# Batch-by-batch keys, choices and digits for the first routing round of a retention, MoE and GLU kernel

## The chip, the cores and the metric

The program runs on one core of one Trainium2 chip. The metric is the device time of one execution in microseconds (us); several executions are timed and the median is taken. The engines of the core work side by side and meet only at semaphores: TensorE (PE, with its weight loads shown apart as PEld), VectorE (DVE), ScalarE (ACT), GpSimd (POOL) and SyncE (SP), which issues the DMA transfers. Each of them takes its own instructions strictly in order.

## The reference

Three layers follow one another. The first is a retention layer over 4 batches, 8 heads, 768 steps and head size 64:

```python
for t in range(S):
    state = gamma[None, :, None, None] * state + np.einsum('bhd,bhe->bhde', k[:, :, t], v[:, :, t])
    y[:, :, t] = scale * np.einsum('bhd,bhde->bhe', q[:, :, t], state)
```

Its output is 3072 tokens of 512 numbers. The second layer sends each token to one of 8 experts with a capacity of 384 tokens each. All logits (token, expert) are walked from the largest down; a token goes to the expert of the first logit whose expert still has room:

```python
logits = x @ w_gate
order = np.argsort(-logits.flatten())
for idx in order:
    tok, e = (int(idx) // E, int(idx) % E)
    if assigned[tok] >= 0 or counts[e] >= cap:
        continue
    assigned[tok] = e
    counts[e] += 1
for e in range(E):
    mask = assigned == e
    h = np.maximum(x[mask] @ w1[e], 0.0)
    out[mask] = h @ w2[e]
```

The third layer is a gated unit on all tokens: `(sigmoid(x @ w_gate) * (x @ w_val)) @ w_out`.

## The kernel before

**Tiling.** The tokens of a batch are cut into C = 6 tiles of 128 (one per partition), so there are U = 24 units, numbered u = 6b + c. The attention part runs as a software pipeline over steps s = 0 to 28. In step s, unit s-1 has q and k transposed (PE lines 648 and 655), unit s-2 its scores made (636) and masked by DVE (`att`, 572), unit s-3 its output and state products (684, 688, 698) and DVE's scaling into `xTa` (584) and the running `state` (594, 597), unit s-4 its partial logits (668) and DVE's transposition into `xrow` (563), and unit s-5 its logits finished on PE (623) and copied by DVE into column u of `logits` (554). Steps 0 to 5 and 24 to 28 are written out; steps 6 to 23 are a hardware loop over b = 1, 2, 3 with six steps in its body, so step s has b = s // 6 and c = s % 6.

**Who waits for whom in a step.** PE's products of line 668 in step s wait until DVE has made the copy of unit s-5, since both use the bank `ps_l`. They are the first thing on PE in a step that needs DVE work of that same step. DVE's `xTa` waits for the products of line 688. ACT copies the transposed q, k and the partial logits (`qT`, `kT`, `lparts`, lines 518, 523, 531).

**The queue of SP.** In step s SP issues the loads of q and k for unit s+5 and of v for unit s+3, and then four stores of `xrow` for unit s-4. From step 19 on four loads of resident weights stand behind each step's stores. From step 21 on ACT has `high` (line 282) for three resident tiles behind each step's copies; the first of a group of four waits until its four loads have landed.

**After the attention.** DVE waits for all logits and then prepares the first routing round: `prepare(True)` finds for each token the best logit (`best`), turns it into a sortable integer (`bits`, `key`), finds the expert it belongs to (`wide`, `top`, `choice`) and cuts the key into seven digits of five bits (`digit_i`, `digit_f`). The arrays have one column per unit. Then a radix search alternates DVE and PE in seven visits (`compare_first`, `first_threshold`), the chosen tokens are numbered, their row numbers go to GpSimd's gather, and the expert rounds begin. Each later round's routing is done beside the matmuls of the round before it.

**Waits within DVE.** `link(ins)` lets DVE wait until ins has written its result; `count_only(ins)` counts it on the same semaphore (`dve_chain`) and goes on at once. `PREP_CHAIN` and `CHAIN_START` are where the count stands before the first round.

Of the kernel before, what the change touches and what calls it, by code (L numbers as in the profile page):

```python
# [8 lines left out]
I32 = mybir.dt.int32  # L9
U32 = mybir.dt.uint32  # L10
ALU = mybir.AluOpType
ACT = mybir.ActivationFunctionType
AX_X = mybir.AxisListType.X
P = 128


def retention_moe_glu_kernel(nc, q, k, v, w_router, w1, w2, w_gate, w_val, w_out, decay, out):
# [15 lines left out]
    with ctx:  # L33
# [21 lines left out]
        BIG = 1.0e6  # L55
        PREP_CHAIN = 13
        FIRST_CHAIN = 79
        ROUTE_CHAIN = 125
        CHAIN_START = PREP_CHAIN
        TABLES = 8 + 5 + 3 + 3  # L60
# [226 lines left out]
        if True:  # L287
# [251 lines left out]

            def attend_vector(dve):  # L540
                nc.vector.memset(state[:, :, :, :], 0.0).then_inc(state_cleared, 1)
# [7 lines left out]
                def body(b, c, s):  # L549
# [25 lines left out]
                    if alive(s, 3):  # L575
# [10 lines left out]
                        if cc < C - 1:  # L586
# [3 lines left out]
                            for half in range(2):  # L590
# [4 lines left out]
                                else:  # L595

                                    ins = nc.vector.tensor_tensor(state[rows, new, :, rows], fresh_kv,
                                                                  state[rows, cc % 2, :, rows], ALU.add)
                                ins.then_inc(state_ready, 1)

                slots(dve, body, 0, U + 4)
# [294 lines left out]
        def _(dve):  # L896
            attend_vector(dve)

            link_count = [0]
# [73 lines left out]

            def prepare(first):
                prepare_keys()
                prepare_digits(first)

# [10 lines left out]

            def prepare_digits(first):

# [6 lines left out]
                link(nc.vector.tensor_scalar(digit_f[:, :, :], digit_i[:, :, :], 1.0, None, ALU.add))  # L997
                if first:
                    compare_first(digit_f[:, 0, :])
                else:  # L1000
                    compare(digit_f[:, 0, :])
                raise_by(digit_f[:, 0, :], 1)
# [164 lines left out]
            def one_round(i, follows):  # L1167
# [21 lines left out]
                def prepare_next():  # L1189

                    if vis[0] == VISITS + 1 and follows:
                        close()
                        prepare_keys()
                        vis[0] += 1
                    elif vis[0] == VISITS + 2 and follows:
                        prepare_digits(False)
                        vis[0] += 1
# [35 lines left out]
                out_rows(i)  # L1233

            dve.sem_inc(orow_ready, TT)
            dve.sem_inc(orow_free, 1)
            dve.wait_ge(tables_made, TABLES)
# [8 lines left out]
            close()  # L1246
            prepare(False)
            assert link_count[0] == FIRST_CHAIN, link_count[0]
# [224 lines left out]
```

## Time and profile before

| what | us |
|---|---|
| median of 3 executions | 1080.89 |
| lowest and highest of them | 1080.59, 1082.13 |
| the profiled execution, its own time | 1084.76 |
| span of the profiled execution, from its first to its last instruction | 1082.7 |
| PE busy in the span | 1027.4 |
| DVE busy in the span | 697.5 |

Times in rows are microseconds from the start of the span. The granted clock (PEclk) is 1.00 at TensorE's 2.4 GHz and 0.50 at 1.2 GHz. A note in brackets behind a row is the idle time of that engine before it and what ended it.

### The profile page before, as it was taken

To read this page: it belongs to the slowest core of one execution; us is meant where nothing else is said; L and a number is where in the kernel's file an instruction comes from. 1 tells how busy PE (TensorE), PEld (TensorE's weight loads), DVE (VectorE), ACT (ScalarE), POOL (GpSimd) and SP (SyncE) were. 2 spreads that over 40 slices of the span, in tenths; PEclk is the share of its full clock that TensorE was granted. 3 is DMA by queue.
4 is the path that set the end of the run, shared out by engine and by line. 5 is a ranking of instruction groups with operands and counts; after the bars stand their busy time and mean duration, and the time that the engine had idled before them with its cause. 6 is when DMAs were issued, how large, how long until landed. Compare 5 with 4: busy or idle time off the path is not lost.

```text
span 1082.7 us, 20008 instructions
## 1 busy us (share of the span) xinstructions
PE 1027.4 (95%) x7130; PEld 958.4 (89%) x7130; DVE 697.5 (64%) x1880; ACT 330.0 (30%) x630; POOL 116.6 (11%) x141
## 2 busy tenths in 40 slices
PE   8999734999999999999999999999999999999996
PEld 7888623999999999999999999999999999999995
DVE  4777578777577657766776677666775677554211
ACT  3222423422333233322332333233412341234110
POOL 4212601033000101010100010011001100110001
PEclk9999865999999999999999999999999999999998
DMA  8899843403241324122322332132314231323000
GB/s 197 202 222 229 224 137 117 119 29 93 74 146 40 88 78 128 59 83 83 110 77 59 107 108 79 49 117 92 95 39 127 80 107 38 119 78 117 1 1 30
DMA packets 197356, 107.69 MB, mean 99 GB/s; under 512 B 81936, under 2 KB 182800, under 8 KB 197264
## 3 DMA queue, kind: packets, MB, share of 16 engines
q1 hardware_dynamic: 193424, 93.94, 31.2%
q0 software_dynamic: 3840, 12.59, 3.6%
q8 instruction: 50, 0.82, 0.3%
q14 instruction: 42, 0.34, 0.1%
HBM read 88.41 MB, written 18.09 MB: 98 GB/s over the span
## 4 chain that ended last, share of the span: by engine, by line
PE 93%; DVE 2%; DMA 1%; issue 1%; SPq 1%; ACT 0%; POOL 0%; DVEq 0%; POOLq 0%; ACTq 0%
PE bank L1323 21%; PE bank L1325 21%; PE bank L1324 21%; PE bank L1416 6%; PE bank L1417 6%; PE bank L1415 6%; PE bank L636 2%; PE bank L688 2%; PE bank L684 2%; PE bank L648 1%; PE bank L1277 1%; PE bank L655 1%; PE bank L698 1%; PE bank L668 1%; PE bank L610 1%
## 5 line engine op out<-in xcount | busy, mean ns | idle before, releaser
L1323 PE MATMUL bank<-h2h,resident 128*128 128x384 f32 x768 | 261.2, 340 | 0.0
L1325 PE MATMUL bank<-h2h,resident 128*128 128x384 f32 x768 | 257.9, 336 | 0.0
L1324 PE MATMUL bank<-h2l,resident 128*128 128x384 f32 x768 | 257.3, 335 | 0.0
L1323 PEld LDWEIGHTS bank<-h2h,resident 128*128 128x128 f32 x768 | 144.4, 188 | 2.9
L1324 PEld LDWEIGHTS bank<-h2l,resident 128*128 128x128 f32 x768 | 144.3, 188 | 2.9
L1325 PEld LDWEIGHTS bank<-h2h,resident 128*128 128x128 f32 x768 | 144.1, 188 | 0.0
L834 ACT ACTIVATE ring<-ring_raw 128x512 fp32r<-128x512 f32 x192 | 117.7, 624 | 61.7 <-DMA ring_raw<-in_moe_w_out_dram 42.0
L1150 DVE TENSOR_TENSOR pf<-bank,gate 128x384 f32<-128x384 f32 x96 | 53.5, 557 | 123.7 <-PE bank L1325 115.9
L858 ACT ACTIVATE ph<-pf 128x384 fp32r<-128x384 f32 x96 | 50.4, 525 | 252.1 <-DVE pf L1150 252.1
L1159 DVE TENSOR_TENSOR ring<-ring_raw,ring 128x512 fp32r<-128x512 f32 x192 | 126.0, 682 | 0.0
L854 ACT ACTIVATE gate<-bank 128x384 f32<-128x384 f32 x96 | 46.9, 489 | 145.9 <-PE bank L1325 145.8
L1154 DVE TENSOR_TENSOR pl<-pf,ph 128x384 fp32r<-128x384 f32 x96 | 54.2, 564 | 56.8 <-ACT ph L858 56.8
L1323 PE MATMUL bank<-xh,ring 128*128 128x384 f32 x256 | 88.4, 345 | 0.6 <-DVE xl L1140 0.6
L1323 PE MATMUL bank<-hh,ring 128*128 128x384 f32 x256 | 87.0, 340 | 0.0
L1324 PE MATMUL bank<-xl,ring 128*128 128x384 f32 x256 | 86.4, 337 | 0.0
L1325 PE MATMUL bank<-xh,ring 128*128 128x384 f32 x256 | 86.3, 337 | 0.0
L1324 PE MATMUL bank<-hl,ring 128*128 128x384 f32 x256 | 85.7, 335 | 0.0
L1325 PE MATMUL bank<-hh,ring 128*128 128x384 f32 x256 | 85.7, 335 | 0.0
L1417 PE MATMUL bank<-ring,pl 128*128 128x512 f32 x192 | 76.0, 396 | 0.0
L1416 PE MATMUL bank<-ring,ph 128*128 128x512 f32 x192 | 75.8, 395 | 0.0
L1415 PE MATMUL bank<-ring,ph 128*128 128x512 f32 x192 | 74.8, 390 | 0.2 <-issue 0.2
L791 POOL DMA_INDIRECT xg<-xrows,ids x24 | 23.4, 977 | 460.2 <-DVE ids L1111 419.1
(192 smaller groups left out, 1642.4 us busy)
## 6 DMA issues: line engine op xcount, KB each, us to landing
ring_raw<-in_moe_w_dram SPq DMA_DIRECT2D x128, 256.0 KB, 3.0
ring_raw<-in_moe_w_out_dram SPq DMA_DIRECT2D x64, 256.0 KB, 2.8
qraw<-in_q_dram SPq DMA_DIRECT2D x24, 256.0 KB, 3.3
kraw<-in_k_dram SPq DMA_DIRECT2D x24, 256.0 KB, 3.7
vraw<-in_v_dram SPq DMA_DIRECT2D x24, 256.0 KB, 4.2
xrows<-xrow SPq DMA_DIRECT2D x96, 64.0 KB, 2.3
xlaid<-xg SPq DMA_DIRECT2D x7, 768.0 KB, 4.4
zg<-xlaid SPq DMA_DIRECT2D x28, 192.0 KB, 4.2
```

The lines of the kernel that those rows point to most:

```text
L834: nc.scalar.activation(ring[:, n % RING, 0, :], ring_raw[n % RING][:, :], ACT.Copy).then_inc(piece_hi, 1)
L854: nc.scalar.activation(gate[:, f % 2, :], bank[2 * (f % 2)][:, 0:CAP], ACT.Sigmoid).then_inc(gate_ready, 1)
L858: nc.scalar.activation(ph[:, f % 2, :], pf[:, f % 2, :], ACT.Copy).then_inc(ph_ready, 1)
L1150: nc.vector.tensor_tensor(pf[:, f % 2, :], bank[2 * (f % 2) + 1][:, 0:CAP], gate[:, f % 2, :], ALU.mult).then_inc(p_ready, 1)
L1154: nc.vector.tensor_tensor(pl[:, f % 2, :], pf[:, f % 2, :], ph[:, f % 2, :].bitcast(F32), ALU.subtract).then_inc(pl_ready, 1)
L1159: nc.vector.tensor_tensor(ring[:, s, 1, :], ring_raw[s][:, :], ring[:, s, 0, :].bitcast(F32), ALU.subtract).then_inc(piece_lo, 1)
L1323: nc.tensor.matmul(ps, wh, xhi, start=start, stop=False)
L1324: nc.tensor.matmul(ps, wh, xlo, start=False, stop=False)
L1325: return nc.tensor.matmul(ps, wl, xhi, start=False, stop=stop)
L1415: nc.tensor.matmul(PS_OUT[j][:, :], ph[:, f % 2, toks], wh, start=f == 0, stop=False)
L1416: nc.tensor.matmul(PS_OUT[j][:, :], ph[:, f % 2, toks], wl, start=False, stop=False)
L1417: last = nc.tensor.matmul(PS_OUT[j][:, :], pl[:, f % 2, toks], wh, start=False, stop=False)
```

## The change

The keys, choices and digits of the first routing round are made in pieces of six columns. For the first three batches DVE makes them inside the attention loop: the six instructions of `first_keys` for batch b-1 stand at the end of the loop's step c = 4, the five of `first_digits` at the end of its step c = 5. Only the fourth batch's six columns remain behind the attention (`prepare_last`). The product of `top` with `unassigned`, which is all ones in the first round, is left out of the first round, so that 11 instructions per batch stand where 12 stood for all batches. Later rounds are prepared as before.

```diff
-        CHAIN_START = PREP_CHAIN
+        UNIT_CHAIN = 11
+        CHAIN_START = (U // C) * UNIT_CHAIN + 1
...
+                    if s is None and c >= C - 2:
+                        prepare_ahead(b, c - C + 2)
...
+            def first_keys(n):
+
+                tiles = bass.ds(n * C, C)
+                logged = masked[:, :, tiles]
+                link(nc.vector.reduce_max(best[:, tiles], over_experts(logged), AX_X))
+                count_only(nc.vector.tensor_scalar(bits[:, tiles], best[:, tiles], 0.0, None, ALU.add))
+                link(nc.vector.tensor_tensor(wide[:, :, tiles], logged, best[:, tiles].unsqueeze(1).to_broadcast([P, E, C]), ALU.is_equal))
+                count_only(nc.vector.tensor_scalar(key[:, tiles], bits[:, tiles].bitcast(I32), 31, -2147483648,
+                                                   ALU.arith_shift_right, ALU.bitwise_or))
+                link(nc.vector.tensor_tensor(wide[:, :, tiles], wide[:, :, tiles],
+                                             priority[:, :].unsqueeze(2).to_broadcast([P, E, C]), ALU.mult))
+                count_only(nc.vector.tensor_tensor(key[:, tiles], key[:, tiles], bits[:, tiles].bitcast(I32), ALU.bitwise_xor))
+
+            def first_digits(n):
+
+                tiles = bass.ds(n * C, C)
+                link(nc.vector.reduce_max(top[:, 0, tiles], over_experts(wide[:, :, tiles]), AX_X))
+                count_only(nc.vector.tensor_tensor(digit_i[:, :, tiles], key[:, tiles].unsqueeze(1).to_broadcast([P, DIGITS, C]),
+                                                   shift[:, :].unsqueeze(2).to_broadcast([P, DIGITS, C]), ALU.logical_shift_right))
+                link(nc.vector.tensor_tensor(choice[:, :, tiles], priority[:, :].unsqueeze(2).to_broadcast([P, E, C]),
+                                             top[:, 0, tiles].unsqueeze(1).to_broadcast([P, E, C]), ALU.is_equal))
+                link(nc.vector.tensor_scalar(digit_i[:, :, tiles], digit_i[:, :, tiles], RADIX - 1, None, ALU.bitwise_and))
+                link(nc.vector.tensor_scalar(digit_f[:, :, tiles], digit_i[:, :, tiles], 1.0, None, ALU.add))
+
+            def prepare_ahead(b, part):
+
+                link_base[0] = (b - 1) * UNIT_CHAIN
+                link_count[0] = 0 if part == 0 else 6
+                if part == 0:
+                    dve.wait_ge(tables_made, TABLES)
+                    dve.wait_ge(logits_saved, b * C)
+                    first_keys(b - 1)
...
+                else:
+                    first_digits(b - 1)
...
+            def prepare_last():
+
+                link_base[0] = 0
+                link_count[0] = (B - 1) * UNIT_CHAIN
+                first_keys(B - 1)
+                first_digits(B - 1)
+                compare_first(digit_f[:, 0, :])
+                raise_by(digit_f[:, 0, :], 1)
...
             dve.wait_ge(logits_saved, U)
-            prepare(True)
+            prepare_last()
```

On DVE, at the end of step c = 4 of the attention loop, the first instructions of `first_keys` come in behind the state update and ahead of the next step's copy of logits. REGISTER_ALU and ISA rows are work of the sequencer: addresses and the counts waited for, which depend on the loop's b.

```order
 L597 TENSOR_TENSOR state<-bank,state 64x4x64
+L978 ISA [waits logits_saved,tables_made]
+L978 TENSOR_REDUCE best<-logits 128x6
+L905 ISA
+L979 REGISTER_ALU [waits dve_chain]
+L979 TENSOR_SCALAR bits<-best 128x6
+L980 REGISTER_ALU
+L980 TENSOR_TENSOR wide<-logits,best 128x8x6
+L905 REGISTER_ALU
+L981 REGISTER_ALU [waits dve_chain]
```

The copy of logits (line 554) stood directly behind the state update; now six vector instructions stand between them. The same happens at the end of step c = 5, where the loop turns. Its last instructions and the branch are these:

```order
+L993 TENSOR_TENSOR choice<-priority,top 128x8x6
+L905 REGISTER_ALU
+L995 TENSOR_SCALAR digit_i<-digit_i 128x7x6 [waits dve_chain]
+L905 REGISTER_ALU
+L996 REGISTER_ALU [waits dve_chain]
+L996 TENSOR_SCALAR digit_f<-digit_i 128x7x6
+L905 REGISTER_ALU
+L358 REGISTER_ALU [waits dve_chain]
 L358 COMPARE_AND_BRANCH
 L554 COPY logits<-bank 128x8 [waits logits_done]
```

The branch now comes behind a wait for the last of the five new instructions. Behind the attention, DVE's preparation of the first round read so before:

```order
-L980 TENSOR_REDUCE best<-logits 128x24 [waits logits_saved,tables_made]
-L981 TENSOR_SCALAR bits<-best 128x24 [waits dve_chain]
-L982 TENSOR_TENSOR wide<-logits,best 128x192
-L984 TENSOR_SCALAR key<-bits 128x24 [waits dve_chain]
-L986 TENSOR_TENSOR wide<-wide,priority 128x192
-L987 TENSOR_TENSOR key<-key,bits 128x24 [waits dve_chain]
-L991 TENSOR_REDUCE top<-wide 128x24
-L992 TENSOR_TENSOR digit_i<-key,shift 128x168 [waits dve_chain]
-L994 TENSOR_TENSOR top<-top,unassigned 128x24
-L995 TENSOR_SCALAR digit_i<-digit_i 128x168 [waits dve_chain]
-L996 TENSOR_TENSOR choice<-priority,top 128x192
-L997 TENSOR_SCALAR digit_f<-digit_i 128x168 [waits dve_chain]
```

and reads so now, in the same place:

```order
+L978 TENSOR_REDUCE best<-logits 128x6 [waits logits_saved]
+L979 TENSOR_SCALAR bits<-best 128x6 [waits dve_chain]
+L980 TENSOR_TENSOR wide<-logits,best 128x8x6
+L981 TENSOR_SCALAR key<-bits 128x6 [waits dve_chain]
+L983 TENSOR_TENSOR wide<-wide,priority 128x8x6
+L985 TENSOR_TENSOR key<-key,bits 128x6 [waits dve_chain]
+L990 TENSOR_REDUCE top<-wide 128x6
+L991 TENSOR_TENSOR digit_i<-key,shift 128x7x6 [waits dve_chain]
+L993 TENSOR_TENSOR choice<-priority,top 128x8x6
+L995 TENSOR_SCALAR digit_i<-digit_i 128x7x6 [waits dve_chain]
+L996 TENSOR_SCALAR digit_f<-digit_i 128x7x6
```

Each instruction there has a quarter of the elements, and one instruction with its wait is gone.

## Rows read from the trace of the kernel before

**Rows 1.** The page, part 4: the chain that ended last, shares by engine.
```profile
PE 93%; DVE 2%; DMA 1%; issue 1%; SPq 1%; ACT 0%; POOL 0%; DVEq 0%; POOLq 0%; ACTq 0%
```

**Rows 2.** Timeline of DVE, preparation of the first round: start, duration, line, tiles.
```profile
139.55 0.62 DVE L980 TENSOR_REDUCE best<-logits 128x24 f32<-128x192 f32 x1
140.20 0.18 DVE L981 TENSOR_SCALAR bits<-best 128x24 f32<-128x24 f32 x1
140.29 0.35 DVE L982 TENSOR_TENSOR wide<-logits,best 128x192 f32<-128x192 f32 x1
...
141.25 0.61 DVE L991 TENSOR_REDUCE top<-wide 128x24 f32<-128x192 f32 x1
141.89 0.33 DVE L992 TENSOR_TENSOR digit_i<-key,shift 128x168 int32<-128x168 int32 x1
142.15 0.17 DVE L994 TENSOR_TENSOR top<-top,unassigned 128x24 f32<-128x24 f32 x1
...
142.90 0.25 DVE L997 TENSOR_SCALAR digit_f<-digit_i 128x168 bf16<-128x168 int32 x1
143.18 0.63 DVE L929 TENSOR_TENSOR above_first<-digit_f,ladder 128x384 bf16<-128x384 bf16 x2
```

**Rows 3.** Timeline of DVE, two short forms in the first round.
```profile
144.92 0.16 DVE L952 TENSOR_REDUCE flag<-reached 128x1 f32<-128x8 bf16 x1
...
167.80 0.20 DVE L1065 TENSOR_TENSOR member_id<-position,member 128x48 bf16<-128x48 f32 x1
```

**Rows 4.** Timeline of DVE: a looped address behind a wait; the loop's branch on DVE's sequencer.
```profile
257.67 0.71 DVE L1111 TENSOR_REDUCE ids<-slot_sums 32x3 uint32<-32x6 f32 x4
258.51 0.17 DVE L1120 COPY ids_all<-ids 128x3 uint32 x1
...
L358 DVEq COMPARE_BRANCH  x3: 50/63/67, 57.4 to 124.1; - x3
```

**Rows 5.** Timeline of all engines, a step of the attention loop (step 18).
```profile
87.97 0.17 DVE L554 COPY logits<-bank 128x8 f32 x1
...
89.24 0.16 PEld L668 LDWEIGHTS bank<-xTa,wr 128*32 128x32 f32 x8 [0.17 <-issue]
...
91.61 0.69 DVE L584 TENSOR_TENSOR xTa<-bank,growth 128x512 f32<-128x512 f32 x1 [1.19 <-PE bank L688]
```

**Rows 6.** Timeline of DVE and PE, a step whose PE waits for the copy (step 26).
```profile
134.41 0.17 DVE L554 COPY logits<-bank 128x8 f32<-128x8 f32 x1
...
134.70 0.19 PEld L668 LDWEIGHTS bank<-xTa,wr 128*32 128x32 f32 x8 [1.15 <-issue]
```

**Rows 7.** Timeline of DVE and PE, the step behind the loop (step 24).
```profile
123.90 0.30 PEld L623 LDWEIGHTS bank<-pick,lparts 128*128 128x128 f32 x2
...
125.06 0.17 DVE L554 COPY logits<-bank 128x8 f32<-128x8 f32 x1
...
126.34 0.16 PEld L668 LDWEIGHTS bank<-xTa,wr 128*32 128x32 f32 x8 [0.17 <-issue]
```

**Rows 8.** Timeline of PE, SP and ACT around PE's longest wait in the attention.
```profile
99.02 0.60 PE L655 MATMUL bank<-ident,ks 128*128 128x128 f32 x4
...
100.18 0.43 SPq L376 DMA_DIRECT2D qraw<-in_q_dram  x1
...
108.78 0.51 SPq L273 DMA_DIRECT2D resident_raw<-in_moe_w_val_dram  x1
...
113.78 1.67 ACT L282 ACTIVATE resident<-resident_raw 128x512 fp32r<-128x512 f32 x3 [8.62 <-DMA resident_raw<-in_moe_w_val_dram]
...
116.64 0.59 PE L623 MATMUL bank<-pick,lparts 128*128 128x8 f32 x2 [5.34 <-ACT lparts L531]
```

**Rows 9.** Busy time by stretch: PE, PEld, DVE, ACT, POOL, clock, DMA share, GB/s.
```profile
111.00:116.60 5.60, 0.30 (x12) 0.16 (x6) 1.32 (x3) 2.82 (x7) 2.11 (x2) 0.82 0.94 246
116.60:121.00 4.40, 4.36 (x26) 3.85 (x26) 2.57 (x4) 1.50 (x3) 3.13 (x4) 0.50 0.97 272
```

**Rows 10.** Timeline of ACT, the copies of step 23.
```profile
122.01 0.28 ACT L531 ACTIVATE lparts<-bank 128x128 f32<-128x128 f32 x1
```

More of the change, by code:

```diff
@@ L55, in retention_moe_glu_kernel @@
         BIG = 1.0e6
-        PREP_CHAIN = 13
         FIRST_CHAIN = 79
         ROUTE_CHAIN = 125
-        CHAIN_START = PREP_CHAIN
+        UNIT_CHAIN = 11
+        CHAIN_START = (U // C) * UNIT_CHAIN + 1
         TABLES = 8 + 5 + 3 + 3
@@ L538, in attend_scalar, with attend_vector @@
                 assert highs[0] == EARLY
-            def attend_vector(dve):
+            def attend_vector(dve, prepare_ahead):
                 nc.vector.memset(state[:, :, :, :], 0.0).then_inc(state_cleared, 1)
@@ L896, in _ @@
         def _(dve):
-            attend_vector(dve)
             link_count = [0]
@@ L972, in threshold @@
                 link(last)
-            def prepare(first):
+            def first_keys(n):
[9 more added lines that the diff above has]
+                count_only(nc.vector.tensor_tensor(key[:, tiles], key[:, tiles], bits[:, tiles].bitcast(I32), ALU.bitwise_xor))
@@ new lines, in prepare_ahead @@
+            def prepare_ahead(b, part):
[5 more added lines that the diff above has]
+                    first_keys(b - 1)
+                    assert link_count[0] == 6
+                else:
+                    first_digits(b - 1)
+                    assert link_count[0] == UNIT_CHAIN
+            def prepare_last():
[5 more added lines that the diff above has]
+                raise_by(digit_f[:, 0, :], 1)
@@ L975, in prepare @@
+            def prepare():
                 prepare_keys()
-                prepare_digits(first)
+                prepare_digits()
             def prepare_keys():
@@ L987, in prepare_keys, with prepare_digits @@
                 count_only(nc.vector.tensor_tensor(key[:, :], key[:, :], bits[:, :].bitcast(I32), ALU.bitwise_xor))
-            def prepare_digits(first):
+            def prepare_digits():
                 link(nc.vector.reduce_max(top[:, 0, :], over_experts(wide[:, :, :]), AX_X))
@@ L997, in prepare_digits @@
                 link(nc.vector.tensor_scalar(digit_f[:, :, :], digit_i[:, :, :], 1.0, None, ALU.add))
[L998 to L1001, printed above, removed]
+                compare(digit_f[:, 0, :])
                 raise_by(digit_f[:, 0, :], 1)
@@ L1195, in prepare_next @@
                     elif vis[0] == VISITS + 2 and follows:
-                        prepare_digits(False)
+                        prepare_digits()
                         vis[0] += 1
@@ L1233, in one_round @@
                 out_rows(i)
+            attend_vector(dve, prepare_ahead)
             dve.sem_inc(orow_ready, TT)
             dve.sem_inc(orow_free, 1)
-            dve.wait_ge(tables_made, TABLES)
             dve.wait_ge(logits_saved, U)
-            prepare(True)
+            prepare_last()
             assert link_count[0] == CHAIN_START, link_count[0]
@@ L1246, in _ @@
             close()
-            prepare(False)
+            prepare()
             assert link_count[0] == FIRST_CHAIN, link_count[0]
```

## The prediction

> **What bounds the kernel now.** I read the shares of the chain that ended last first: 93% of it is PE [rows 1]. DVE's 2% lie mostly between the end of the attention and the first expert round, where PE has nothing to do but the small products of the search. So the change can gain in that stretch and nowhere else, and it can lose wherever its new work comes to hold up PE inside the attention. The timeline of DVE gives the first: from the start of `best` at 139.55 to the start of `above_first` at 143.18 the preparation takes 3.63 us, one instruction after the other, with all other engines waiting for it [rows 2]. The timeline of a step gives the second: DVE is idle for only 1.19 us in a step of 5.15 us (the step from one `xTa` to the next), ahead of `xTa` [rows 5]. And the timeline around PE's longest wait in the attention, 5.34 us ahead of step 23, shows what released it: ACT stood at `high` until the fourth resident load, issued at 108.78, landed at about 113.7, then made its copies, and PE went on at 116.64 [rows 8].
>
> **What goes behind the attention.** The sizes needed are between rows. A two-input operation takes 0.35 on 192 elements, 0.20 on 48, and 0.17 to 0.18 on 24 [rows 2, 3]; so 0.20 for the new 48-element forms. The reduce over experts takes 0.62 for 192 elements and the smallest 0.16 for 8 [rows 2, 3]; a straight line between them gives 0.26 for 48, taken as 0.27 for its strided read. The digit operations have 168 elements at 0.33 and 0.25, 42 now: 0.20 and 0.18. A `link` adds 0.03 (`best` ends at 140.17, `bits` starts at 140.20), and an instruction behind `count_only` starts 0.09 after it (140.20 to 140.29) [rows 2]. First half: 0.30 for `best`, 0.09, 0.23, 0.09, 0.23, 0.09, sum 1.03. Second half: 0.30 for `top`, 0.11 for the shift, 0.23, 0.21, 0.21, sum 1.06. Together 2.09 in place of 3.63: **1.54 saved**, 0.20 of it from the product with `unassigned` (142.15 to the next start). Bounds: were the small forms as cheap as the smallest rows (0.16 for a reduce, 0.17 to 0.18 for the rest), the sum is 1.77 and 1.86 is saved; were they as dear as the full-size rows, only the 0.20 is saved. I take 1.54, since the 48-element row is of exactly the new size. What comes behind (search, numbering, gather) follows DVE's chain and moves up by as much; the resident loads that run beside it are issued earlier and are not waited for there.
>
> **What comes into the loop.** The same instructions, with work of the sequencer added. Where an address depends on the loop and stands behind a wait, the copy into `ids_all` shows the price: `ids` ends at 258.38 and the copy starts at 258.51, 0.13 in place of 0.03 [rows 4]. Each half has two such places, 0.20 together, and one register operation between two instructions without a wait, for which I put 0.04, between nothing and that 0.10. The second half ends in a wait with a register operation and the branch, 0.06 for the branch [rows 4] and 0.04 for the operation. So the first half delays what follows by 1.27 and the second by 1.40. With the cheap and dear rows the second half is 1.23 or 2.46 (the first 1.12 or 2.3).
>
> **Who waits for it.** Behind each half stands the copy of logits, and PE's products of line 668 wait for that copy. Where they do wait for it, they start 0.29 after the copy's start (134.41 to 134.70) [rows 6]. In a normal step the copy starts at 87.97 and the products at 89.24, 1.27 later [rows 5], so 0.98 is slack. A first half costs PE 1.27 - 0.98, about 0.3, and a second 0.4. Nothing else in the step is nearer: the masks `att`, `xTa` and `state` come up to 1.4 later, but DVE's idle 1.19 ahead of `xTa` takes that up, together with PE's own shift. The transposed rows come later too, but SP stores them two steps behind. Registers aside no other queue changes.
>
> The halves stand behind steps 10, 11, 16, 17, 22 and 23. The first four push PE by 0.3, 0.4, 0.3 and 0.4, **1.4 in all**, ahead of the 5.34 us wait. I cost them at nothing. What hides them is the wait on ACT, and what sets its end is SP's queue and the transfers, which do not follow PE: SP issues the last q load, of unit 23, at 100.18, in its step 18, while PE transposed unit 19, in its step 20, at 99.02 [rows 8]. SP is two steps behind PE and needs nothing that PE is late with. If that cover were gone, they would cost 1.4. The fifth, behind step 22, falls inside that wait. The sixth, behind step 23, has no cover: there the copy starts at 125.06 and the products at 126.34 [rows 7], slack 0.99, so PE is **pushed by 0.41**, and every later step with it, since PE and DVE hand over to each other to the end (at 134.41 PE waits for the copy outright [rows 6]). Bounds 0.24 and 1.47.
>
> **Sum.** -1.54 + 0.41 = -1.13, so -1.1 us. The profiled execution would go from 1084.76 to 1083.7, its span from 1082.7 to 1081.6. That execution stands 3.9 above the median of the runs; the difference is carried over to the median as it is: 1080.9 - 1.1 = 1079.8. Cheap forms give -1.86 + 0.24 = -1.6, dear ones -0.20 + 1.47 = +1.3.
>
> A rule of the skill speaks against such a change. The rows say that 24 columns cost 0.35 and six cost 0.20 for a two-input operation, so four pieces take 0.80 of DVE in place of 0.35. The Trainium skill has this as a rule (VectorE: DVE Perf Modes, section on the TRN2 errata): operations on SBUF pay a fixed latency per instruction, and many small tiles pay it each time. It would count all of DVE's time: three batches at 1.27 + 1.40 put 8.0 into the loop, and if DVE bound the attention the sum would be about +6.5. The trace disagrees with that, DVE being idle 1.19 in a step.
>
> **Rivals.** *The clock stays up.* In the wait of 5.34 us the granted clock falls: it is 0.82 over 111.0 to 116.6 and 0.50 (1.2 GHz) over 116.6 to 121.0, when PE is busy again [rows 9]. With PE arriving 1.4 later, the wait is 3.9 us. If that is too short for the fall, PE does the work up to line 668 of step 23 in 2.4 (123.90 to 126.34, the same work in step 24 [rows 7]) in place of 4.4. Not all of that 2.0 is kept: in step 24 PE's first product needs ACT's `lparts`, made from 122.01 to 122.29 behind a load that does not move [rows 10], so it starts at 122.5 in place of 123.9 and 1.4 are won. Result -2.5, 1078.4. For it: PE arrives late in the same stretch. Against it: 3.9 us is still a long wait. The Trainium skill (TensorE: Matmul & The Clock Gate, part 1) has the clock held down by idle time and released by activity, on a beat that runs free of the kernel; by that rule the same wait can end either way from one execution to the next, and a shorter one falls less often. I give it a chance of 0.25.
>
> *The cover is missing.* If the end of the 5.34 us wait moves with PE, because SP is tied to PE after all (its loads of q wait for PE's transpositions), the 1.4 comes back and the result is +0.3, 1081.2, slower than before. It decides from the point at which SP is less than PE's delay behind, and the two steps (10 us) speak against it. Chance 0.10.
>
> *Small pieces cost as much as whole ones.* If six strided columns take what 24 take, the last half's push is 1.47 and the gain 0.2: +1.3, 1082.2. It decides where the push exceeds 1.54 less what is not saved; the 48-element row at 0.20 speaks against it. Together with a missing cover four more pushes of 1.3 to 1.5 would make it +7, past 0.2%. Chance 0.10, of which 0.05 past 0.2%.
>
> *It does less than it says* would need the preparation to be hidden behind something now; the other engines' idleness at 139.55 to 143.18 excludes it.
>
> **How the numbers follow.** Forecast 1079.8 with 0.55, clock 0.25, cover 0.10, dear pieces 0.10. A measurement of this kernel can tell about 0.2%, 2.2 us, from no change. The forecast and the cover rival lie within it, the clock rival at -2.5 lies just past it and I count 0.2 of its 0.25 as faster. So faster 0.20, same 0.74, slower 0.06. The range reaches from the clock rival to nearly the dear pieces, 1078.2 to 1082.0, and leaves out under 0.2.
>
> **What would show it.** In the trace after: about 2.1 us from the last batch's `best` to `above_first` in place of 3.63; the copy of logits 1.3 to 1.4 later against the state update in steps 11, 12, 17, 18 and 24 and PE's line 668 waiting 0.3 to 0.4 for it there; PE's wait ahead of step 23 shorter by the same sum and ending at 116.6 as before; the granted clock behind it at 0.50. It is wrong if that wait ends later than 116.6, if the pushes are above 1 us, or if the clock there reads 1.00.

## The result

Five runs of each kernel, side by side, gave a median of 1090.96 us for the changed kernel (1088.55 to 1093.31) and 1080.64 for the kernel before (1078.68 to 1082.13). The ratio is 1.0094, with a 95% interval of 1.0077 to 1.0112. The change makes the kernel 10 us slower, where 1.1 faster was predicted, and outside the range given. The profiled execution of the changed kernel took 1090.21 (span 1088.2, before 1082.7). The two profiled executions differ by 5.5 and the medians by 10.3, since that of before stands 4.1 above the median of these five runs and that of the changed kernel 0.8 below its own; what the wait in the profile of before has to do with it comes up below.

The preparation behind the attention did what was worked out. Timeline of DVE, changed kernel, the fourth batch (line numbers are up to 43 higher than before):

```profile
138.97 0.27 DVE L978 TENSOR_REDUCE best<-logits 128x6 f32<-128x48 f32 x1
139.28 0.17 DVE L979 TENSOR_SCALAR bits<-best 128x6 f32<-128x6 f32 x1
139.36 0.20 DVE L980 TENSOR_TENSOR wide<-logits,best 128x48 f32<-128x48 f32 x1
...
141.07 0.63 DVE L929 TENSOR_TENSOR above_first<-digit_f,ladder 128x384 bf16<-128x384 bf16 x2
```

From `best` to `above_first` are 2.10 us (predicted 2.09) in place of 3.63 [rows 2]. The first round ends earlier too: PE's first product of the first expert starts at 179.97, where before it started at 182.19:

```profile
179.97 0.66 PE L1366 MATMUL bank<-xh,ring 128*128 128x384 f32 x1 [0.63 <-DVE xl L1183]
```
```profile
182.19 0.66 PE L1323 MATMUL bank<-xh,ring 128*128 128x384 f32 x1 [0.62 <-DVE xl L1140]
```

So in these two executions the loss lies wholly behind it, in code that the change does not touch. From that product to the end of the span are 1088.2 - 179.97 = 908.2 us, before 1082.7 - 182.19 = 900.5: 7.7 lost. The chain of waits says where to look. Its shares by engine, to be read against [rows 1], where DVE had 2% and issue 1%:

```profile
PE 88%; DVE 6%; issue 4%; DMA 1%; DVEq 0%; ACT 0%; POOL 0%; POOLq 0%
```

The list of waits of the changed kernel (engine, tile and line, who releases it: us in total, times, longest) names it:

```profile
DVE short L964 <- issue: 15.5, 6, 2.9
DVE hl L1171 <- ACT hh L848: 11.3, 10, 1.5
DVE short L962 <- issue: 9.7, 6, 1.8
PEld bank L1366 <- DVE hl L1171: 7.3, 6, 1.6
```

The kernel before has the second and the third of these (10.8, 9 times, and 9.5, 6 times) and neither the first nor the last. The six times are the six turns of DVE's loop over the experts. "issue" means that DVE waited for nothing the trace shows. Timeline of DVE at one turn, changed kernel, and the same place before:

```profile
297.49 0.15 DVE L962 TENSOR_TENSOR short<-room,bank 32x8 f32<-32x8 f32 x1 [1.59 <-issue]
297.68 0.15 DVE L964 TENSOR_TENSOR short<-short,bank 32x8 f32<-32x8 f32 x1
300.08 0.16 DVE L964 TENSOR_TENSOR short<-short,bank 32x8 f32<-32x8 f32 x1 [2.25 <-issue]
300.27 0.16 DVE L965 TENSOR_TENSOR reached<-short,bank 32x8 bf16<-32x8 f32 x1
```
```profile
299.16 0.15 DVE L962 TENSOR_TENSOR short<-room,bank 32x8 f32<-32x8 f32 x1 [1.71 <-issue]
299.35 0.34 DVE L964 TENSOR_TENSOR short<-short,bank 32x8 f32<-32x8 f32 x2
```

Behind the turn DVE stands 1.6 to 1.8 us in both kernels, which nobody waits for. In the changed kernel it makes two vector instructions and stands again, 2.6 us on average, so that `hl` comes too late for PE: 7.3 us in all, nearly the whole 7.7.

The attention was not as predicted either. These are PE's weight loads of line 670 (668 before) behind each half; a normal step has 0.17 there [rows 5]:

```profile
56.20 0.19 PEld L670 LDWEIGHTS bank<-xTa,wr 128*32 128x32 f32 x8 [0.53 <-issue]
62.99 0.19 PEld L670 LDWEIGHTS bank<-xTa,wr 128*32 128x32 f32 x8 [1.74 <-issue]
87.80 0.19 PEld L670 LDWEIGHTS bank<-xTa,wr 128*32 128x32 f32 x8 [0.52 <-issue]
93.87 0.19 PEld L670 LDWEIGHTS bank<-xTa,wr 128*32 128x32 f32 x8 [1.06 <-issue]
118.67 0.19 PEld L670 LDWEIGHTS bank<-xTa,wr 128*32 128x32 f32 x8 [0.52 <-issue]
125.80 0.19 PEld L670 LDWEIGHTS bank<-xTa,wr 128*32 128x32 f32 x8 [2.12 <-issue]
```

With 0.17 taken off, the first halves push PE by 0.35 or 0.36 each (predicted 0.3), the second halves by 1.57, 0.89 and 1.95 (predicted 0.4): 5.5 us together where 2.1 had been worked out (1.4 ahead of the long wait, 0.3 inside it, 0.4 behind). That this did not show in the start of the first expert's products has two reasons, both at the wait of [rows 8]. PE did not wait there at all (line 625 started at 115.88, without an idle time), and the clock behind it stayed at 1.00. Busy time by stretch of the changed kernel, columns as in [rows 9]:

```profile
111.00:116.60 5.60, 5.60 (x90) 5.00 (x91) 4.22 (x10) 3.33 (x7) 4.18 (x4) 1.00 0.95 255
116.60:121.00 4.40, 4.08 (x68) 3.56 (x68) 3.79 (x11) 3.21 (x7) 3.32 (x4) 1.00 1.03 302
```

### The profile page after: what moved, and what is told of

Same layout as the page of the kernel before. It is cut to its first block, busy times and chain, and to the rows that moved or that the text cites. A ratio compares the mean times of both kernels' runs of the same rounds, so it can differ in the third digit from the quotient of the medians.

```text
span 1088.2 us, 20087 instructions
## 1 busy us (share of the span) xinstructions
PE 1029.2 (95%) x7130; PEld 958.5 (88%) x7130; DVE 703.9 (65%) x1912; ACT 330.6 (30%) x630; POOL 116.7 (11%) x141
## 4 chain that ended last, share of the span: by engine, by line
PE 88%; DVE 6%; issue 4%; DMA 1%; DVEq 0%; ACT 0%; POOL 0%; POOLq 0%
PE bank L1366 20%; PE bank L1368 19%; PE bank L1367 19%; PE bank L1459 6%; PE bank L1460 6%; PE bank L1458 6%; PE bank L690 2%; PE bank L686 2%; PE bank L638 2%; PE bank L650 1%; PE bank L1320 1%; PE bank L670 1%; DVE orow L1208 1%; PE bank L612 1%; PE bank L657 1%
```

## First experiments: where the expert loop's code lies

DVE's expert loop is a loop in its program too. Counted in the compiled program, its first instruction is DVE's 293rd (counted from 0) before and the 318th in the changed kernel; the body has 372. The trace shows DVE's code arriving: small transfers on queue q14, 43 of them with 0.34 MB in the changed kernel, so 8 KB each. I took an instruction as 64 bytes, which makes 128 instructions of such a transfer; the version with 128 increments below tests that. My theory was that the added 25 instructions moved the head of the loop to the very end of such a block, so that DVE, having jumped back, soon runs out of code and waits for the next block, which it has only begun to fetch. In the program's order the second instruction of line 964, the one that DVE stands ahead of, is the sixth of the loop; of the five ahead of it two are the vector instructions that it makes and three are work of the sequencer. The rival is that the halves themselves (their registers, their state, what they do to SP's and ACT's queues) slow the later rounds. The edit that separates them adds increments of a semaphore that nobody waits for, ahead of the attention loop. They do no work; what they change is the place of what follows, and DVE's start by the time that they take:

```diff
                 nc.vector.memset(state[:, :, :, :], 0.0).then_inc(state_cleared, 1)
+                for _ in range(25):
+                    dve.sem_inc(padding, 1)
```

> The kernel before with 25 such increments ahead of the attention loop on DVE, which puts its expert loop at the same place in DVE's code (instruction 318) as in the changed kernel; the work is that of before. Theory placement: line 964 waits about 2.6 us at each turn of the loop and the time rises by 8 to 10 us, to about 1090, although no work is changed. Rival, the new work itself: no change, 1080.7.

> The kernel before with 33 increments, eight more than x_before_pad25. Theory placement: the expert loop starts just behind a boundary, line 964 does not wait, and the time is that of before, 1080.7 within 1 us. Rival, that added instructions ahead of the loop cost by their number: at least as slow as x_before_pad25.

> The changed kernel with eight increments of an unused semaphore on DVE ahead of its attention loop, where DVE waits for other work anyway; all work is done as before. In the trace of the changed kernel, at each of the six turns of the expert loop that are followed by routing, the second line-964 instruction stands still for about 2.6 us with no releaser, right behind a transfer of the instruction queue. Theory placement: the loop's first instructions lie at the end of a block of fetched code; eight instructions more put them behind that boundary, the wait at line 964 goes, and PE's wait for hl at the start of each round (7.3 us in all) with it: about 1078.5, slightly faster than before, since the expert rounds start 2.2 us earlier. Rival: the loss comes from the new work itself (other transfers, later resident weights, larger counts on the chain): about 1091, as the changed kernel. Rival of my prediction, that the attention part loses: 1083 or more.

| kernel | loop begins at | median us (runs) | ratio to before, 95% | first expert's product to end |
|---|---|---|---|---|
| before | 293 | 1080.55 (29) | 1 | 900.5 |
| before, 25 increments | 318 | 1086.77 (6) | 1.0055, 1.0035 to 1.0076 | 905.9 |
| before, 33 increments | 326 | 1080.57 (12) | 1.0003, 0.9991 to 1.0016 | 898.7 |
| after, no increments (from the result above) | 318 | 1090.96 (5) | 1.0094, 1.0077 to 1.0112 | 908.2 |
| after, 8 increments | 326 | 1083.21 (12) | 1.0030, 1.0019 to 1.0042 | 898.7 |

The kernel before, with 25 increments and no other change, is 6.2 us slower (8 to 10 had been expected), and its list of waits has the same entries as the changed kernel's, at the same places:

```profile
DVE short L967 <- issue: 14.0, 6, 3.3
...
DVE short L965 <- issue: 9.7, 6, 1.8
PEld bank L1326 <- DVE hl L1131: 5.8, 6, 2.1
```

Eight increments more take all of it away again in both kernels. This settles the larger part: of the changed kernel's loss of 10.3 us, 7.7 come from the place of the expert loop's code by the medians (1090.96 to 1083.21), and the stretch lost as much against before (908.2 to 900.5). The size is less sure than the cause: in the unchanged work the same place cost 6.2 by the medians and 5.4 in the stretch, from 6 runs. The rest, 2.6 us, is what the change does in the attention. With it the version with 8 increments missed its expected 1078.5; it came out at the 1083 of the rival for the attention.

Two more places ask what kind of boundary it is.

> The changed kernel with 128 semaphore increments of DVE ahead of its attention loop, so that DVE's expert loop begins at its instruction 446 in place of 318: 128 further on. The transfers of DVE's code seen in the trace are of 128 instructions. If what is lost in the expert rounds depends on where the loop begins within such a block of 128, this version loses as much as the changed kernel: about 1091, with issue waits of 2.5 to 3 us in DVE at the turn of the loop. If blocks are of 256 instructions, or the loss hangs on the distance from the start of the program, it goes like the version with 8 increments: about 1083, without those waits.

> The changed kernel with 4 semaphore increments of DVE ahead of its attention loop: the expert loop of DVE begins at instruction 322, between 318 (loses some 8 us) and 326 (does not). If the loss comes from a block of code that ends a few instructions behind the head of the loop, so that DVE runs out of fetched instructions there, the end lies between 318 and 326 and this version either loses as much as 318 (about 1091, the end still inside the loop's first instructions) or nothing (about 1083). If the loss grows and falls evenly with the place, it is half, about 1087.

With 128 increments (loop at 446) the median was 1094.51, 1.0115 of before (1.0095 to 1.0136), and the entry is back (group of instructions: busy us, mean ns | idle before and its releaser):

```profile
L967 DVE TENSOR_TENSOR short<-short,bank 32x8 f32<-32x8 f32 x98 | 15.2, 155 | 18.0 <-issue 14.9
```

With 4 increments (loop at 322) it was 1083.55, 1.0014 of a before of 1082.19 beside it (1.0003 to 1.0026), without the entry. The two good places of the changed kernel thus stand 1.4 and 2.7 us above the runs beside them, so what is left for the attention is known to about a microsecond. So the bad place comes back after 128 instructions, the size of one transfer, and its edge lies between 318 and 322: four instructions decide over some 7 us. (The 128 increments themselves also delay DVE's start by some 4 us, which is why this version is slower than the changed kernel: its first expert's product starts at 185.81 and 906.7 follow.)

The Trainium skill tells of this (Runtime: NRT & Kernel Launch, section on instruction fetch mechanics): prefetch of code is purely sequential, and a taken branch whose target is not in the window stalls the engine while the target is fetched. The runs agree with that. The page gives the blocks as 16 KiB, 256 instructions, and the window as two of them; by that size the version with 128 increments would have been free of the wait. For DVE the transfers are of 8 KB and the bad place repeats with 128 (so does the good one, 293 and 421 below), so here the measurement decides.

One row of the page of the profile says more than I looked for: the transfers of DVE's code in the whole execution (packets, MB, share). The changed kernel, then the same with 8 increments:

```profile
q14 instruction: 43, 0.34, 0.1%
```
```profile
q14 instruction: 12, 0.10, 0.0%
```

Kernels whose loop begins at 322 or 326 fetch 12 blocks; all with other places (293, 318, 421, 446) 42 to 44, some five per turn more. In the former the waits at the loop's first line are gone as well; those of the kernel before (9.5 us) were hidden, and their absence gains nothing that shows: with 4 increments the stretch is 900.4, before 900.5. The 898.7 of two versions in the table is of another kind. In them PE's clock read 1.00 from the first expert's product on, where before it read 0.50 for its first 4 us, and a version whose loop begins at 421, with 9.6 us of these waits (the control below), has 1076.8 - 178.04 = 898.8 with the same clock. Their first product, here of the version with 33 increments and then of the control, takes 0.41 in place of 0.66:

```profile
177.87 0.41 PE L1326 MATMUL bank<-xh,ring 128*128 128x384 f32 x1 [0.62 <-DVE xl L1143]
```
```profile
178.04 0.41 PE L1326 MATMUL bank<-xh,ring 128*128 128x384 f32 x1 [0.62 <-DVE xl L1143]
```

A body of 372 instructions from 322 or 326 ends at 694 or 698. If a block begins at 322, that is three blocks, and from 318 or 293 it is four. That three stay in DVE's memory and four do not fits all kernels (the body has 371 instructions in the versions with two batches), but no run tested another length of body.

## Second experiments: what is left in the attention

Two explanations stood for the remaining 2.6 us: the halves' place behind the state update, where the copy of logits and with it PE wait for them; or something else that makes them long. The first try moved the halves ahead of DVE's wait for `xTa`, where it is idle 1.19 us in a step [rows 5]:

```diff
+                    if s is None and c >= C - 2:
+                        prepare_ahead(b, c - C + 2)
                     if alive(s, 3):
...
                         dve.wait_ge(y_done, u + 1)
...
-                    if s is None and c >= C - 2:
-                        prepare_ahead(b, c - C + 2)
```

> x_after_pad8 with the halves moved from the end of their steps to the place ahead of xTa, where DVE is idle 1.2 us in each step. Theory: DVE's copy of logits is no longer delayed by them, so PE's waits at line 670 (0.35, 1.57, 0.35, 0.89 and about 1.9 us in the changed kernel) fall to 0.3 or less; in exchange PE reaches its wait for ACT earlier and may see the clock fall there again. Between 1077 and 1079.5. If the pushes cost nothing because they are covered: the same as x_after_pad8.

It took 1082.15 (12 runs), 1.0011 of before (0.9996 to 1.0026), 1.1 below the version with the halves in their old place, whose interval overlaps with this one, and above the 1079.5 expected at most. Four of the six pushes were gone from its trace, and two remained: PE's weight loads waited 1.13 and 2.99 us in steps 23 and 24, the latter longer than any before. DVE and POOL there:

```profile
110.86 0.24 DVE L981 TENSOR_REDUCE best<-logits  x1
111.23 1.10 DVE L982 TENSOR_SCALAR bits<-best  x1
112.24 0.20 DVE L983 TENSOR_TENSOR wide<-logits,best  x1
112.56 1.03 DVE L984 TENSOR_SCALAR key<-bits  x1
113.50 0.20 DVE L986 TENSOR_TENSOR wide<-wide,priority 128x48 f32 x1
113.73 1.12 DVE L988 TENSOR_TENSOR key<-key,bits  x1
```
```profile
111.02 5.04 POOL L276 TENSOR_TENSOR resident<-resident_raw,resident 128x512 fp32r<-128x512 f32 x4 [8.36 <-ACT resident L282]
```

POOL makes the low parts of the resident weights, four subtractions of 1.26 us one behind the other, so they end at about 112.3, 113.5, 114.8 and 116.1. The three long operations of DVE, on six columns and 0.17 us long elsewhere, end at 112.33, 113.59 and 114.85: each waited out POOL's current operation. The changed kernel has the same in step 23, beside POOL's stretch of five subtractions from 118.49 to 124.71, the fourth of which ends at about 123.5:

```profile
122.96 0.59 DVE L991 TENSOR_TENSOR digit_i<-key,shift 128x42 int32 x1
123.47 1.30 DVE L993 TENSOR_TENSOR choice<-priority,top 128x48 f32 x1
```

and in step 11, where `digit_f` (61.21, 0.82 us) ends as POOL's `ks` (60.94, 1.05 us) does. Both fit, with ends at 123.55 and 124.77. The first two batches can meet POOL only at a single `ks` in a step; the third meets the resident weights, which are made there. In the traces of the changed kernel and of its version with 8 increments, each time one of the third batch's two halves met them. In the latter one more thing follows. PE's weight load waited 2.57, and the clock fell behind it (columns as in [rows 9]):

```profile
118.00:120.00 2.00, 0.07 (x4) 0.10 (x8) 1.93 (x5) 0.45 (x1) 1.56 (x2) 1.00 1.04 295
120.00:122.00 2.00, 2.00 (x24) 1.80 (x26) 1.91 (x3) 1.58 (x4) 0.71 (x1) 0.58 0.98 277
122.00:124.00 2.00, 2.00 (x30) 2.00 (x28) 0.03 (x1) 0.25 (x1) 2.00 (x3) 0.56 0.99 286
```

So a long push can cost more than itself. To test that POOL is the cause, POOL's subtraction was replaced by a store, in the changed kernel and in the one before alike, both with the expert loop at 326:

```diff
-            nc.gpsimd.tensor_tensor(resident[:, r, 1, :], resident_raw[r][:, :], resident[:, r, 0, :].bitcast(F32),
-                                    ALU.subtract).then_inc(resident_lo, 1)
+            nc.gpsimd.memset(resident[:, r, 1, :].bitcast(F32), 0.0).then_inc(resident_lo, 1)
```

> The changed kernel with 8 increments (DVE's expert loop where no time is lost), and with POOL's subtraction for the low parts of the resident weights replaced by a store of zeros, which reads nothing from SBUF; so the low parts are left out of the products. Theory: of the 2.6 us by which the version with 8 increments stands above before with 33, most is DVE's small operations of the third batch held up while POOL subtracts (each lasts until POOL's current subtraction of 1.25 us ends). Then none of the small operations of steps 22 to 24 lasts over 0.35 us here, PE's first product of line 670 behind each half waits 0.35 and 0.9 us, not 2.1 to 2.6, and this kernel is at most 0.5 us above, or below, the kernel before with the same replacement. Rival: the small operations are long because of transfers or of PE, and stay at 1.0 to 1.3 us; the difference stays at 2.6 us.

> The kernel before with 33 increments (DVE's expert loop at the same instruction as in the changed kernel with 8), and with POOL's subtraction for the low parts of the resident weights replaced by a store of zeros; the low parts are left out of the products. It is the partner of the changed kernel with the same replacement. By the theory of POOL it is some 0 to 1 us faster than before with 33 increments (1080.6), since its own operations on two SBUF tensors are rare in that stretch; the changed one stands within 0.5 us of it. By the rival the changed one stands 2.6 us above it.

Measured: after 1080.75 (11 runs), before 1081.25 (12 runs). With POOL's subtraction the changed kernel stands 2.6 us above (1083.21 and 1080.57), without it 0.5 below. The mean granted clock of the runs was 0.9758 in both of the first pair, 0.9764 and 0.9747 in the second, so a part of these 3.1 may be the clock's, and the two pairs were not run side by side; among the runs at 0.977 alone the changed kernel is 3.4 above with the subtraction (1082.5 and 1079.1, 3 and 6 runs) and equal without (1080.0 and 1080.0, 3 each). Beside the same runs of before as the second pair (1082.19), the version with 4 increments stands 1.4 above with the subtraction. The operations of step 22 read 0.17 to 0.27 now, and of step 23 only one is long, 0.50, beside a store of POOL:

```profile
117.40 0.17 DVE L983 TENSOR_SCALAR key<-bits  x1
...
122.87 0.21 DVE L995 TENSOR_TENSOR choice<-priority,top 128x48 f32 x1
123.11 0.50 DVE L997 TENSOR_SCALAR digit_i<-digit_i  x1
```

The expectation was missed in two points: that 0.50, and a wait of 1.41 ahead of PE's line 672 in step 17, where a first half's `key` lasted 1.05 us from 85.94 on, beside a `ks` of POOL of 1.04 from 85.94 on:

```profile
87.32 0.19 PEld L672 LDWEIGHTS bank<-xTa,wr 128*32 128x32 f32 x8 [1.41 <-issue]
```

So POOL's operations are the cause of the long operations, in the second batch too. That they are the cause of what the third batch's halves cost fits the times, but is less strictly shown: in that trace PE waited for ACT ahead of both halves' products (0.58 and 0.73), which would have covered a part of their delay in any case. The Trainium skill names the mechanism (SBUF — State Buffer, section on who interferes with whom): DVE and GpSimd share a pair of ports as an exclusive lock, which a DVE operation needs in a two-port mode, or with two SBUF inputs beside a GpSimd operation that reads SBUF, and whichever starts first holds it for its whole instruction. The trace agrees, with ends that match to 0.1 us, and adds how it falls on small operations: 0.17 us of work waits up to 1.1 for a port.

## Third experiments: a version without the third batch

If that is right, the third batch should not be prepared in the loop. Its steps belong to the loop's last turn, so DVE's last six steps were written out, once with the halves of all three batches where they were, once with the third batch joined to the fourth behind the attention, in pieces of 12 columns:

```diff
-                slots(dve, body, 0, U + 4)
+                slots(dve, body, 0, U + 4, unrolled=2)
...
-                first_keys(B - 1)
-                first_digits(B - 1)
+                first_keys(B - 2, 2)
+                first_digits(B - 2, 2)
```

> The changed kernel with the last six steps of DVE's attention loop written out, the halves of all three batches at the same steps as in the changed kernel, and 32 increments, so that DVE's expert loop begins at instruction 421, the same place in a block of 128 as in the kernel before (293). It is the partner of the next one. By the theory of placement: no issue waits of 2.9 us at the expert loop's turn; by the theory of POOL the third batch's halves still hold PE up by 2 to 3 us together. Time as the version with 8 increments, 1083 to 1084 beside a before of 1081 to 1082.

> As its partner with the last six steps written out, but the third batch is prepared with the fourth behind the attention, in pieces of 12 columns, so that no small operation of DVE stands in steps 22 and 23, where POOL subtracts; the expert loop begins at instruction 421 as well. Theory of POOL: the waits of 2.1 to 2.6 us and of 0.5 us ahead of PE's line 670 in steps 23 and 24 are gone, the stretch behind the attention takes 2.4 in place of 2.1 us, and the time is 2 to 3 us below the partner's. Rival: the pushes are made up elsewhere, by a wait for ACT or by the clock, and the two differ by less than 0.5.

> As the version with two batches in the loop, but with each half ahead of DVE's wait for the values of xTa, where DVE is idle 1.19 us in a step, in place of behind the state update. If the four remaining pushes of 0.35 and 0.9 us are what is left, this takes 1 to 2 us more off, ending at or below the kernel before; if they are hidden by ACT's wait for its load anyway, it equals the version with two batches to within 0.5.

> The kernel before with the last six steps of DVE's attention loop written out, as in the version with two batches in the loop, and 70 increments, so that DVE's expert loop begins at instruction 421 as there; the preparation is all behind the attention, as before. It is the control for that version, which took 0.9978 of before. If its gain is of the preparation's move, this one stands at 1.000 of before (within 0.001), and its runs scatter over mean granted clocks of 0.972 to 0.977 as before's do, where those of the version with two batches lie at 0.977. If the gain is of the written-out steps, this one stands at 0.998 as well.

| kernel, expert loop at 421 | median us (12 runs each) | ratio to before, 95% | mean granted clock of the runs |
|---|---|---|---|
| three batches in the loop | 1082.51 | 1.0004, 0.9993 to 1.0015 | 0.9761 |
| two batches | 1080.54 | 0.9978, 0.9966 to 0.9990 | 0.9769 |
| two batches, halves ahead of `xTa` | 1083.01 | 1.0010, 0.9997 to 1.0023 | 0.9735 |
| none (control) | 1081.85 | 1.0004, 0.9987 to 1.0020 | 0.9754 |
| before, beside the first three | 1082.37 (29 runs) | 1 | 0.9743 |

Two batches are 2.0 us faster than three, as expected, and the pushes of steps 23 and 24 are gone. Three batches in this form were a miss: they equal the kernel before (1083 to 1084 beside 1081 to 1082 had been expected), where the looped forms with 4 and 8 increments were 1.4 and 2.7 above it. With two batches the stretch behind the attention takes 2.59 us (136.13 to 138.72), 0.5 more than with one batch. This is the only version with all of the work whose interval lies below the kernel before, by 0.22%. The control, at 1.0004 beside another 17 runs of before, speaks against a part of the written-out steps in it; the two intervals just overlap, and by the medians alone the control stands 1.3 above this version.

The third row was a miss. The version with hardly a push (0.43 in step 12, none elsewhere) should have been the best, and it equals the kernel before. The last column suggests why: its runs had the lowest mean clock. Busy time by stretch, two batches in the old place and then ahead of `xTa`:

```profile
111.00:116.60 5.60, 5.60 (x95) 5.02 (x92) 4.21 (x9) 3.33 (x7) 4.53 (x4) 1.00 1.01 286
116.60:121.00 4.40, 4.40 (x74) 3.82 (x72) 3.16 (x6) 3.32 (x7) 3.22 (x4) 1.00 1.00 288
```
```profile
111.00:116.60 5.60, 2.40 (x48) 2.25 (x45) 1.68 (x5) 3.33 (x7) 2.64 (x3) 1.00 0.95 260
116.60:121.00 4.40, 4.40 (x42) 3.65 (x44) 2.50 (x4) 2.27 (x6) 3.87 (x4) 0.61 1.05 304
```

With hardly a push PE comes to the wait for ACT early, stands 3.19 us, and afterwards works at a granted clock of 0.61, near the lower level of 1.2 GHz; with pushes of 0.36, 1.51, 0.35 and 0.46 on the way it does not wait there at all and stays at 2.4 GHz. Over all runs of the control, those with a mean clock of 0.977 took 1079.6 on average and those with 0.974 took 1083.1. Of the version with two batches 11 in 12 had 0.977, averaging 1080.1. My reading is that the pushes fall into a wait, and by shortening it spare the slow clock that some executions of the kernel before pay for. At an equal clock of 0.977 this version is no faster than before's runs with that clock, whose means in the four groups of runs were 1079.7 to 1080.7 (1080.1 beside it, as its own). So there the 1.05 us less of preparation do not show, and the pushes may have eaten them up. That the clock is the cause and not a companion was not tested by itself; the sizes fit roughly: 0.0015 more mean clock than the control are 1.6 us of a span of 1080, the preparation gives at most 1.05 (3.64 to 2.59), together at most 2.7, and 0.26% or 2.8 us were measured by the ratios.

One number of this set sizes the turn of the attention loop. At the second batch's second half the written-out version leaves the loop, where the changed kernel jumps back. The weight load behind it waits 0.63 in the one and 1.06 in the other (a part of that can be the address of the copy of logits, which depends on the loop's b only where the steps are looped):

```profile
93.38 0.19 PEld L673 LDWEIGHTS bank<-xTa,wr 128*32 128x32 f32 x8 [0.63 <-issue]
```

## Why the prediction was wrong

*Preparation behind the attention, 1.54 saved.* Right to 0.01: 2.10 us against 2.09. The short forms were 0.27, 0.17, 0.20 and 0.18 as taken.

*"Registers aside no other queue changes."* This is the step that failed. I counted what the 25 added instructions of DVE execute, and not that they lie ahead of the expert loop in its program. The term was missing altogether, and it is +7.7 of the result (6.2 in the kernel before, with nothing but the place changed). It was not in the trace of before as a cost, only as a harmless sign: 9.5 us of "issue" waits at six turns of the loop, which I did not ask about since nobody waited for them.

*First halves, 0.3.* Right: 0.35.

*Second halves, 0.4.* Too small. The 0.10 for the loop's end with a wait ahead of the branch was 0.64 (`digit_f` ends at 92.94, the copy starts at 93.58), because I took the 0.06 that the branch instruction lasts for what jumping back costs. That makes 0.89 where nothing else is in the way. In two of three cases a POOL operation came on top, 1.57 and 1.95.

*Dear pieces.* I gave this rival 0.10, with the price of whole-size rows. Pieces were cheap, as the row of 48 elements said, and yet the push of step 24 was 1.95, more than its upper bound of 1.47. That bound does not follow from the rows either: `top` to `above_first` takes 1.93 in [rows 2], less the 0.20 left out and with the loop's 0.34 that is 2.07, not 2.46, a push of 1.08. The mechanism, POOL's lock, was not among my cases: I read DVE's rows and not POOL's beside them.

*Cover, 1.4 hidden by PE's wait of 5.34.* Right in kind, wrong in size. The length of that wait differs from one execution to the next: the profiles of four versions of the kernel before that differ only by increments, written-out steps or POOL's operation have 3.27, 1.66, 2.88 and 1.45 there, since the resident load lands between 110.8 and 112.4 in them and at 113.8 in the profile of before. The pushes ahead of it were 3.2, not 1.4, and it ended earlier in the changed kernel's execution.

*Clock rival.* It came true (1.00 in place of 0.82 and 0.50), and by the two profiles the changed kernel's first expert does start 2.2 us earlier, near my -2.5. By the medians there is no such gain. Of the four other profiles the clock fell behind the waits of 3.27 and 2.88 (0.68 in the former over 116.6 to 121.0) and stayed at 1.00 behind those of 1.66 and 1.45; so a part of the executions of before has no slow stretch that the change could undo, and the changed kernel's version with 8 increments has one of its own. That the rival came true in the profiled pair is in part luck. It carried a chance of 0.25 and was worth little beside a term of +7.7 that stood nowhere.

In sum: -1.54 for the preparation, +4.1 for pushes and what they do to waits and clock, and +7.7 for the code's place make the 10.3 measured. The 4.1 is no measurement of its own but what the 2.6 left requires; by the version with 4 increments it is 2.9.

## What to carry to other kernels

An edit that adds instructions moves every later loop in that engine's program. Look at the idle time put down to "issue" at the turns of the loops behind it, count where the loop's head falls among the code transfers, and if the time jumps, try a few idle instructions ahead of the loop before judging the edit. Keep in mind that the next edit moves it again. Work put into an engine's slack must be held against what its neighbour at the shared port does in that stretch, and a wait that is to hide it should be read in more than one execution.

## What the runs showed of the hardware

- DVE's code arrived in transfers of 8 KB, and a bad place of a loop's head came back 128 instructions further on (318 and 446, not 293, 322, 326 or 421). At a bad place DVE stood another 2.3 to 2.6 us at each turn, and the kernel lost 6 to 8 us; four or eight instructions further on it lost none of that, and the transfers fell from 43 to 12.
- A DVE operation of 0.17 to 0.20 us lasted 0.6 to 1.3 us while POOL ran an operation on two SBUF tensors, ending when POOL's operation ended, and 0.50 beside a POOL store.
- The turn of a short loop behind a wait cost 0.64 us, 0.43 more than leaving it, where the branch itself is shown with 0.06.
- A version with delays of 2.7 us ahead of a wait took 2.5 us less than the same with 0.4 us of them. In the profile of the former PE did not stand there and its clock stayed at 1.00; in that of the latter it stood 3.19 us and read 0.61 afterwards. That this is the cause was not tested by itself.
